# Routed experts turned around: weights stationary, highs and lows of 192 tokens as 384 moving columns

## The chip, the core and the metric

One core of a Trainium2 chip runs the whole program. The metric is device time in microseconds (us) of one execution.

## What is computed

The reference is a chain of three layers in fp32, all in one kernel:

```python
attn = softmax_causal(q k^T / 8 + min(bias, 0)) v        # 2 x 8 heads, 576 tokens, 64 wide
x = attn as 1152 rows of 512
e = argmax(x @ w_gate)                                   # layer 2: one of 8 experts for each row
out[row] = gate[row] * (relu(x[row] @ w1[e]) @ w2[e])    # w1 512x1024, w2 1024x512
out2 = sum over 4 experts of p[:, e] * (relu(out @ u1[e]) @ u2[e])   # layer 3: every row, all 4
```

With these inputs the eight experts of layer 2 get 130, 137, 129, 143, 151, 156, 117 and 189 of the 1152 rows.

## The kernel before

Every large product is made from fp32r operands in three passes: an operand is split into a high part (an fp32r copy, written by ScalarE) and a low part (the fp32 value minus the high), and the sum is high by high, high by low and low by high (`PASSES`). Attention (to 141 us) comes first, then routing, the routed experts (the stage that the change rewrites), a gather, and the dense experts of layer 3.

**Routing.** VectorE makes the one-hot, ranks and slots (L769 to L809). Each expert's rows start at a multiple of 128 in `x_slots` in DRAM. GpSimd scatters the rows there with ten indirect DMAs (L457), reading `slot_of`. Meanwhile TensorE runs 16 matmuls of no use (`keep_clock_wide`, L1091) and makes the first tile directly from `x_nat` with selection matrices (L1101), so that tile does not wait for the scatter.

**Routed stage.** The tile is 128 rows, so the counts above make 15 tiles: two for each expert and one for the expert with 117 rows. In `tile` on TensorE (L1104 to L1153) the tokens are the stationary operand and a weight row of 512 columns moves: 24 matmuls up (L1118), 8 transposes of `h1` (L1126), 24 matmuls down (L1135) and 4 transposes of the next tile's rows (L1085). ScalarE takes ReLU and writes the high parts, VectorE the low parts, scales by the gate (L858), and SyncE stores the tile to `y_slots` (L359).

**Splitting the weights.** The weights of the next expert are split while this one runs. They come in eight pieces of 128 x 1024 through four stages (SyncE, L190); ScalarE writes `w_hi` (L584), VectorE `w_lo` of pieces 0, 1, 2, 4, 5, 6 (L838), and GpSimd that of 3 and 7 (L466). Each stage is loaded again when its low part is done. What orders all of this is each engine's program, in which it stands as it is written.

**Gather and dense stage.** After the last store GpSimd gathers the rows back in token order (L477), TensorE transposes them (L1176) and the others write `x2T` high and low; 6 of the 10 row blocks are transposed inside the first dense expert. Then come 4 experts x 3 chunks of 384 tokens (L1191 up, L1206 down), VectorE adds to `acc` (L910), and SyncE stores `acc` (L390).

Of the kernel before, what the change touches and what calls it, by code (L numbers as in the profile page):

```python
# [26 lines left out]
F32 = mybir.dt.float32  # L27
F32R = mybir.dt.float32r
# [9 lines left out]
NT = 5  # L38
# [26 lines left out]
MAXTILES = N // P  # L65
# [4 lines left out]
def moe_chain_kernel(nc, q, k, v, s, wg, w1, w2, dp, u1, u2, out):  # L70
    x_slots = nc.dram_tensor("x_slots", ((SLOT_TILES + 1) * P, XROW), F32, kind="Internal").ap()
    y_slots = nc.dram_tensor("y_slots", (SLOT_TILES * P, DM), F32, kind="Internal").ap()
# [6 lines left out]
    with ExitStack() as ctx:  # L79
# [10 lines left out]
        gate_now = sb("gate_now", [P, 1], F32)  # L90
# [9 lines left out]
        with ExitStack() as a:  # L100
# [4 lines left out]
            thresholds = sb("thresholds", [P, E1, MAXTILES - 1], F32, a)  # L105
# [37 lines left out]

        with ExitStack() as b:
            x_slot = sb("x_slot", [P, XROW], F32, b)
            xT = [sb(f"xT{c}", [P, KD, P], F32R, b) for c in "hl"]
            h1 = [sb(f"h1_{i}", [P, 512], F32, b) for i in range(2)]
            h1T = [[sb(f"h1T{i}{c}", [P, 4, P], F32R, b) for c in "hl"] for i in range(2)]
            y_sb = sb("y_sb", [P, DM], F32, b)


        x2T = [sb(f"x2T{c}", [P, KD, N], F32R) for c in "hl"]

        acc = sb("acc", [P, RT, DM], F32)
        x2_nat = acc
# [10 lines left out]
            slots_zeroed wg_loaded r_step ex_done onehot_ready rank_ready route_ready first_ready scattered  # L166
            hi_done x_slot_loaded xT_psum xT_hi xT_lo h1_ready relu_done h1T_psum h1T_hi h1T_lo y_ready
            y_scaled y_stored gate_copied y_all_stored x2T_psum x2T_hi x2T_lo h2_psum h2_hi h2_lo y2_ready
            y2_added acc_cleared p2_loaded p2_step out_stored passed y_zeroed pads_zeroed""".split()
# [5 lines left out]

        gathered = [sem(f"gathered{r}") for r in range(RT)]
# [26 lines left out]
        X2_AT = 4  # L203
        X2_WITH = (range(0, 4), range(4, 7), range(7, RT))

        def x2_bank(r):

            return (half[3], bank[2], bank[3], half[0], half[3], bank[2], bank[3], half[3], bank[2], bank[3])[r]
# [57 lines left out]
        def _(sp):  # L266
# [35 lines left out]
            sp.wait_ge(m["consts"], 15)  # L302
# [26 lines left out]
            sp.dma_start(x_slots.rearrange("(t p) c -> p t c", p=P),  # L329
                         zeros[:, :].unsqueeze(1).to_broadcast([P, SLOT_TILES + 1, XROW])).then_inc(m["slots_zeroed"], 16)  # L330

            sp.dma_start(y_slots[LEAST_TILES * P:, :].rearrange("(t p) c -> p t c", p=P),
                         zeros[:, 0:DM].unsqueeze(1).to_broadcast([P, SLOT_TILES - LEAST_TILES, DM])).then_inc(m["y_zeroed"], 16)
            sp.dma_start(p2[:, :, :], dp.rearrange("(t p) e -> p t e", p=P)).then_inc(m["p2_loaded"], 16)
# [9 lines left out]
            sp.wait_ge(m["route_ready"], 2)  # L344
            sp.wait_ge(m["scattered"], 16 * RT)
            sp.dma_start(x_slot[:, :], x_slots[0:P, :]).then_inc(m["x_slot_loaded"], 16)
            sp.wait_ge(m["y_zeroed"], 16)
            sp.sem_inc(m["y_stored"], 16)
            T = sp.alloc_register("sp_tile")
            sp.reg_mov(T, 0)  # L350

            def tile(ge=None, e=None, pieces=(), dense=False):

                t = sp.snap(T, min_val=0, max_val=SLOT_TILES - 1)
                sp.wait_ge(m["gate_copied"], t + 1)
                sp.dma_start(x_slot[:, :], x_slots[bass.ds(t * P + P, P), :]).then_inc(m["x_slot_loaded"], 16)
                stream(ge, e, pieces[:2], dense)
                sp.wait_ge(m["y_scaled"], t + 2)
                sp.dma_start(y_slots[bass.ds(t * P, P), :], y_sb[:, :]).then_inc(m["y_stored"], 16)  # L359
                stream(ge, e, pieces[2:], dense)  # L360
                sp.reg_add(T, T, 1)

            def expert(e, after, after2):


                tile(after[0], after[1], W2S, after[2])
                tiles = sp.value_load(tiles_of[0:1, bass.ds(e, 1)], min_val=1, max_val=MAXTILES)
# [878 lines left out]
```

## Time and profile before

| | |
|---|---|
| median of the timed runs | 790.42 us (788.16, 792.26, 790.42) |
| the profiled execution | 785.49 us, its span 783.3 us |
| granted TensorE clock over the span | 0.989 |
| busy: TensorE, VectorE, ScalarE, GpSimd | 747.8, 321.3, 278.6, 159.7 us |
| routed tiles, from the first matmul to the last | 164.5 to 361.8 us |
| gather and first transposes, to the first dense matmul | 361.8 to 375.6 us |
| dense experts to the end | 375.6 to 783.3 us |

Times in the trace are counted from the start of the span. The busy time of TensorE is a sum of overlapping, modelled durations; the pace of matmuls is read from the distance between their starts.

### The profile page before, as it was taken

The page shows a single profiled execution, that of the slowest core. Times are in us where ns is not written, and L with a number is a line of the kernel's source. Part 1 is how long each engine was busy: PE and PEld are TensorE (multiplying, and loading weights), DVE is VectorE, ACT ScalarE, POOL GpSimd, SP SyncE. Part 2 cuts the span into 40 slices and gives each one's busy share as a digit, 9 for nine tenths or more (in the row PEclk, how much of TensorE's full clock was granted, in tenths as well). Part 3 has the DMA queues.
Part 4 walks back from the last instruction along what each step waited for, and adds up shares of the span by engine and source line. Part 5 has one row for each costly group of instructions (what it writes and reads, how often), then busy time and mean ns, then how long its engine had stood idle before and what let it go on. Part 6 is the DMA issues. An engine that isn't in the chain of part 4 may idle for free.

```text
span 783.3 us, 13131 instructions
## 1 busy us (share of the span) xinstructions
PE 747.8 (95%) x4424; PEld 643.5 (82%) x4425; DVE 321.3 (41%) x800; ACT 278.6 (36%) x620; POOL 159.7 (20%) x174
## 2 busy tenths in 40 slices
PE   6999999799999999979899999999999999999998
PEld 5778777578888778767789999999998989999897
DVE  3777777524545455643452314322133211212122
ACT  3777777034545555543332112311113111111110
POOL 4665675222122121223310000110001100000000
PEclk9999999899999999989999999999999999999999
DMA  7744529246575666666530001310012000001011
GB/s 189 213 109 129 159 71 360 83 130 225 181 240 184 220 204 223 198 219 227 162 108 28 1 1 54 120 41 0 0 28 80 0 0 0 0 0 40 0 40 40
DMA packets 61490, 84.35 MB, mean 108 GB/s; under 512 B 33136, under 2 KB 33136, under 8 KB 60944
## 3 DMA queue, kind: packets, MB, share of 16 engines
q1 hardware_dynamic: 59808, 77.95, 31.7%
q0 software_dynamic: 1472, 4.76, 1.9%
q10 hardware_dynamic: 176, 1.22, 0.4%
q8 instruction: 18, 0.29, 0.1%
q14 instruction: 16, 0.13, 0.1%
HBM read 68.82 MB, written 15.09 MB: 107 GB/s over the span
## 4 chain that ended last, share of the span: by engine, by line
PE 69%; issue 20%; POOL 5%; DMA 2%; SPq 1%; DVE 1%; ACT 1%; POOLq 0%; DVEq 0%; ACTq 0%
PE bank L1191 26%; PE wide L1206 25%; PE bank L1051 4%; POOL w_lo L466 3%; PE bank L1033 3%; PE wide L985 3%; PE bank L1016 2%; DMA stages<-in_moe_w 1%; PE wide L1118 1%; POOL x_slots L457 1%; PE bank L1135 1%; PE wide L990 1%; PE wide L959 1%; SPq L276 1%; DMA acc<-y_slots,slot_of 0%
## 5 line engine op out<-in xcount | busy, mean ns | idle before, releaser
L466 POOL TENSOR_TENSOR w_lo<-stages,w_hi 128x1024 fp32r<-128x1024 f32 x22 | 56.9, 2588 | 379.4 <-ACT w_hi L584 379.4
L1191 PE MATMUL bank<-x2Th,w_hi 128*128 128x384 f32 (+1 forms) x384 | 129.3, 337 | 1.6 <-DVE x2Tl L889 1.6
L1191 PE MATMUL bank<-x2Tl,w_hi 128*128 128x384 f32 (+1 forms) x384 | 129.4, 337 | 0.0
L1191 PE MATMUL bank<-x2Th,w_lo 128*128 128x384 f32 (+1 forms) x384 | 128.9, 336 | 0.0
L584 ACT ACTIVATE w_hi<-stages 128x1024 fp32r<-128x1024 f32 x88 | 89.3, 1051 | 5.0 <-DMA stages<-in_moe_w 5.0
L634 ACT ACTIVATE h_0h<-bank 128x384 fp32r<-128x384 f32 x48 | 23.6, 492 | 188.1 <-PE bank L1191 188.1
L838 DVE TENSOR_TENSOR w_lo<-stages,w_hi 128x1024 fp32r<-128x1024 f32 x66 | 79.7, 1227 | 17.3 <-ACT w_hi L584 16.3
L899 DVE SCALAR_TENSOR_TENSOR h_0l<-bank,h_0h 128x384 fp32r<-128x384 f32 x48 | 26.8, 557 | 142.0 <-ACT h_0h L634 142.0
L899 DVE SCALAR_TENSOR_TENSOR h_1l<-bank,h_1h 128x384 fp32r<-128x384 f32 x48 | 26.7, 557 | 129.1 <-ACT h_1h L634 129.1
L1191 PEld LDWEIGHTS bank<-x2Th,w_hi 128*128 128x128 f32 x384 | 72.1, 188 | 5.5 <-issue 1.9
L1191 PEld LDWEIGHTS bank<-x2Th,w_lo 128*128 128x128 f32 x384 | 72.1, 188 | 3.6
L634 ACT ACTIVATE h_1h<-bank 128x384 fp32r<-128x384 f32 x48 | 23.6, 492 | 140.6 <-PE bank L1191 140.6
L1191 PEld LDWEIGHTS bank<-x2Tl,w_hi 128*128 128x128 f32 x384 | 72.0, 188 | 0.0
L446 POOL TENSOR_TENSOR bias<-cum_bc,cum_col 64x64 f32<-64x64 f32 (+4 forms) x80 | 57.0, 720 | 41.8 <-ACT probs L531 33.9
L1206 PE MATMUL wide<-w_lo,h_0h 128*128 128x512 f32 x144 | 57.0, 396 | 0.0
L1206 PE MATMUL wide<-w_hi,h_0l 128*128 128x512 f32 x144 | 56.9, 395 | 0.0
L1206 PE MATMUL wide<-w_lo,h_1h 128*128 128x512 f32 x144 | 56.7, 394 | 0.0
L1206 PE MATMUL wide<-w_hi,h_1l 128*128 128x512 f32 x144 | 56.6, 393 | 0.0
L1206 PE MATMUL wide<-w_hi,h_1h 128*128 128x512 f32 x144 | 56.2, 390 | 0.0
L1206 PE MATMUL wide<-w_hi,h_0h 128*128 128x512 f32 x144 | 56.0, 389 | 0.0
L1118 PE MATMUL wide<-w_hi,xTh 128*128 128x512 f32 x120 | 48.2, 402 | 2.0 <-DVE xTl L829 1.5
L1118 PE MATMUL wide<-w_hi,xTl 128*128 128x512 f32 x120 | 49.4, 412 | 0.0
(190 smaller groups left out, 1331.6 us busy)
## 6 DMA issues: line engine op xcount, KB each, us to landing
stages<-in_moe_w SPq DMA_DIRECT2D x96, 512.0 KB, 3.8
x_slots<-zeros SPq DMA_DIRECT2D x1, 4420.0 KB, 15.4
x_slot<-x_slots SPq DMA_DIRECT2D x16, 260.0 KB, 3.5
y_slots<-y_sb SPq DMA_DIRECT2D x15, 256.0 KB, 2.6
cum_bc<-cum_dram SPq DMA_DIRECT2D x3, 1152.0 KB, 9.1
out_x<-acc SPq DMA_DIRECT2D x9, 256.0 KB, 2.1
q_nat<-in_q SPq DMA_DIRECT2D x16, 128.0 KB, 2.6
k_nat<-in_k SPq DMA_DIRECT2D x16, 128.0 KB, 4.2
```

The source lines that it names most:

```text
L446: g.tensor_tensor(bias[u % BIASES][0:R, 0:K], cum_bc[0:R, bass.ds((4 * odd + 2 * pl + hh) * S, K)], cum_col[0:R, i, bass.ds(it * 4 + (2 * ...
L466: g.tensor_tensor(w_lo[par][:, c], stage[3][:, :], w_hi[par][:, c].bitcast(F32), ALU.subtract).then_inc(lo_done[3], 1)
L584: sc.activation(w_hi[par][:, u * PIECE:(u + 1) * PIECE], stage[u % 4][:, :], ACT.Copy).then_inc(m["hi_done"], 1)
L634: sc.activation(h2[ft % 2][0][:, :], bank[ft % 2][:, 0:CHUNK], ACT.Relu).then_inc(m["h2_hi"], 1)
L838: ve.tensor_tensor(w_lo[par][:, c], stage[u % 4][:, :], w_hi[par][:, c].bitcast(F32), ALU.subtract).then_inc(lo_done[u % 4], 1)
L899: ve.scalar_tensor_tensor(out=h2[ft % 2][1][:, :], in0=bank[ft % 2][:, 0:CHUNK], scalar=0.0, in1=h2[ft % 2][0][:, :].bitcast(F32), op0=ALU ...
L985: te.matmul(wide[hh][0:R, at:at + a1 - a0], qT[pl][st][rows, c0:c0 + R], kT[pl][mv][rows, a0:a1], start=(n == 0), stop=False, skip_group_c ...
L1033: last = te.transpose(dst, pr[0:R, j * P:(j + 1) * P], ident[0:R, 0:R])
L1051: last = te.matmul(bank[2 + u % 2][h_ * D:(h_ + 1) * D, 0:R], v_nat[pl][:, j, h_ * D:(h_ + 1) * D], pT[h_][u % 2][:, j * R:(j + 1) * R], s ...
L1118: last = te.matmul(half[c], xT[st][:, kk, :], w1_of((w_hi, w_lo)[mv][par], kk, c * 512, 512), start=(n == 0), stop=(n == 11))
L1191: last = te.matmul(bank[ft % 2][:, 0:CHUNK], w1_of((w_hi, w_lo)[st][par], kk, ft * P, P), x_mv, start=(n == 0), stop=(n == 11))
L1206: last = te.matmul(half[o], h2[f % 2][st][:, o * P:(o + 1) * P], w2_of((w_hi, w_lo)[mv][par], f), start=(f == 0 and n == 0), stop=(f == KF ...
```

## The change

- **Weights stationary.** A tile is 192 tokens (`TOK`). Its highs and lows stand side by side in `xT[:, kk, 2, 192]`. For each 128 x 128 block of weights one matmul has the high block stationary and 384 columns moving (highs, then lows), and one has the low block stationary and the 192 highs moving. The product comes out transposed, `h1` with its hidden units on partitions, so `h1` isn't transposed.
- **The two halves are added by VectorE**, with a `tensor_reduce` over a pair 192 columns apart in PSUM: eight of 192 outputs for `h1` and two of 384 outputs for the result in each tile.
- **ScalarE** writes the high of ReLU into `h1T`; **GpSimd** writes ReLU in full and then the low.
- **Splits** stand between these: ScalarE splits piece `ft` behind the ReLU of step `ft`, VectorE piece `ft` behind the sum of step `ft`, GpSimd piece 3 in quarters behind steps 3 to 6 and piece 7 behind step 7.
- **Compact slots.** An expert's rows start where those of the one before end (`off_of`); a tile of 192 may run into the next expert's rows, and its result there is written over by the next tile. With these counts there are 8 tiles.
- **Results stay on chip**, in slot order, as highs and lows in `x2T`; `y_slots`, the gather and its transposes go. The gate is folded into `p2`. The token number and the probabilities travel with the row, and the output is scattered by GpSimd with nine indirect DMAs instead of stored by SyncE.
- **The first tile** is loaded from `x_slots` like the others; 80 matmuls of no use stand ahead of it instead of 16.

```diff
+TOK = 192
+LAG = 3
+RAW = 4
...
@@ tensor
-            keep_clock_wide(16)
-            for r in range(RT):
-                pe.wait_ge(m["first_ready"], r + 1)
...
+            keep_clock_wide(80)
+            turn_x(0)
...
+                def up(ft):
+                    if e is not None and ft == 0:
+                        for kk in range(KD):
                             pe.wait_ge(lo_done[kk], e * 2 + 1)
+                    pe.wait_ge(m["h1_sum"], t * KF + (ft + 1))
+                    for kk in range(KD):
+                        te.matmul(up_bank(ft), w1_of(w_hi[par], kk, ft * P, P), xT[:, kk, :, :].rearrange("p a k -> p (a k)"),
+                                  start=(kk == 0), stop=False, skip_group_check=True)
+                        last = te.matmul(up_bank(ft)[:, 0:TOK], w1_of(w_lo[par], kk, ft * P, P), xT[:, kk, 0, :],
+                                         start=False, stop=(kk == KD - 1), skip_group_check=True)
...
+                for ft in range(KF):
+                    up(ft)
+                    if ft >= LAG:
+                        down(ft - LAG)
+                turn_x(t + 1)
+                for f in range(KF - LAG, KF):
+                    down(f)
@@ vector
+                for ft in range(KF):
+                    dve.wait_ge(m["h1_psum"], t * KF + (ft + 1))
+                    dve.wait_ge(m["h1_lo"], t * KF + (ft + 1))
+                    ve.tensor_reduce(h1[:, ft % RAW, :], up_bank(ft).rearrange("p (a k) -> p k a", a=2), AX.X,
+                                     ALU.add).then_inc(m["h1_sum"], 1)
+                    if split is not None and ft % 4 < 3:
+                        split_lo(*split, ft)
+                x_lo(t + 1)
+                for pr in range(2):
+                    dve.wait_ge(m["x2_psum"], t * 2 + (pr + 1))
+                    ve.tensor_reduce(y1[:, 2 * pr:2 * pr + 2, :], down_pair(pr), AX.X, ALU.add).then_inc(m["x2_sum"], 1)
+                for pr in range(2):
+                    dve.wait_ge(m["x2_hi"], t * 2 + (pr + 1))
+                    ve.tensor_tensor(x2T_part(1, pr, col), ...)
@@ scalar
+                for ft in range(KF):
+                    act.wait_ge(m["h1_sum"], t * KF + (ft + 3))
+                    sc.activation(h1T[:, ft % (LAG + 1), 0, :], h1[:, ft % RAW, :], ACT.Relu).then_inc(m["h1_hi"], 1)
+                    if split is not None and ft < KF - 1:
+                        split_hi(*split, ft)
+                x_hi(t + 1)
+                if split is not None:
+                    split_hi(*split, KF - 1)
@@ gpsimd, in the loop over ft
+                    g.tensor_scalar(r1[:, ft % 2, :], h1[:, ft % RAW, :], 0.0, None, ALU.max).then_inc(m["h1_relu"], 1)
...
+                    g.tensor_tensor(h1T[:, ft % (LAG + 1), 1, :], r1[:, ft % 2, :], h1T[:, ft % (LAG + 1), 0, :].bitcast(F32),
+                                    ALU.subtract).then_inc(m["h1_lo"], 1)
...
+                pool.indirect_dma_start(out[:, :], bass.IndirectOffsetOnAxis(token_of[:, t:t + 1], 0),
+                                        acc[:, t, :], None).then_inc(m["out_stored"], 16)
```

How the instructions stand now, at the two places of which the prediction speaks most. First VectorE, in a routed tile, before the change (`h1T..l` and `xTl` are low parts, `w_lo` the low weights of the next expert):

```order
L846 TENSOR_TENSOR h1T0l<-bank,h1T0h 128x512 [waits h1T_hi]
L838 TENSOR_TENSOR w_lo<-stages,w_hi 128x1024 [waits hi_done]
L846 TENSOR_TENSOR h1T1l<-bank,h1T1h 128x512 [waits h1T_hi]
L852 TENSOR_TENSOR xTl<-wide,xTh 128x512 [waits xT_hi]
L838 TENSOR_TENSOR w_lo<-stages,w_hi 128x1024 [waits hi_done]
L838 TENSOR_TENSOR w_lo<-stages,w_hi 128x1024 [waits hi_done]
L858 TENSOR_SCALAR y_sb<-bank,gate_now 128x512 [waits gate_copied,y_stored]
```

And VectorE in the changed kernel, the first three of eight steps of a tile and then the tile's end (`h` is `h1`, `y` is `y1`):

```order
L883 TENSOR_REDUCE h<-bank 128x192 [waits h1_psum,h1_lo]
L873 TENSOR_TENSOR w_lo<-stages,w_hi 128x1024 [waits hi_done]
L883 TENSOR_REDUCE h<-bank 128x192 [waits h1_psum,h1_lo]
L873 TENSOR_TENSOR w_lo<-stages,w_hi 128x1024 [waits hi_done]
L883 TENSOR_REDUCE h<-bank 128x192 [waits h1_psum,h1_lo]
...
L890 TENSOR_REDUCE y<-wide 128x384 [waits x2_psum]
L890 TENSOR_REDUCE y<-wide 128x384 [waits x2_psum]
L893 ISA [waits x2_hi]
L893 TENSOR_TENSOR x2Tl<-y,x2Th 128x2x192
```

Where one weight split stood between three pieces of a tile's own work, a split now stands behind each of six sums, so the next sum is issued only when the split ahead of it has been.

Second ScalarE in the changed kernel, the first steps of a tile:

```order
L661 ACTIVATE h1T<-h 128x192 [waits h1_sum]
L654 ACTIVATE w_hi<-stages 128x1024 [waits stage_full0]
L661 ACTIVATE h1T<-h 128x192 [waits h1_sum]
L654 ACTIVATE w_hi<-stages 128x1024 [waits stage_full1]
L661 ACTIVATE h1T<-h 128x192 [waits h1_sum]
L654 ACTIVATE w_hi<-stages 128x1024 [waits stage_full2]
```

Before, each ReLU was followed by a copy of its transpose, and a split stood alone between them or three together at the tile's end; now each high of the weights stands behind a ReLU that waits for VectorE's sum.

## Rows read from the trace of the kernel before

**Rows 1.** Windows: busy us (x instructions) of PE, PEld, DVE, ACT, POOL; clock; DMA; GB/s.
```profile
164.50:327.90 163.40, 163.23 (x780) 130.85 (x781) 83.67 (x103) 88.11 (x118) 32.18 (x12) 1.00 0.62 200
```

**Rows 2.** Chain of waits, routed stage (start us, us, what).
```profile
177.11 2.67 POOL w_lo L466
...
189.64 2.67 POOL w_lo L466
```

**Rows 3.** Timeline of TensorE: dense matmuls (384 columns), then fp32 transposes (128).
```profile
773.47 0.34 PE L1191 MATMUL bank<-x2Th,w_lo 128*128 x1
773.64 0.34 PE L1191 MATMUL bank<-x2Tl,w_hi 128*128 x1
...
64.87 0.27 PE L959 MATMUL wide<-ident,q_nat 128*128 128x128 f32 x1
64.98 0.27 PE L960 MATMUL wide<-ident,k_nat 128*128 128x128 f32 x1
```

**Rows 4.** Groups by line and form: the splits.
```profile
L584 ACT ACTIVATE w_hi<-stages 128x1024 fp32r<-128x1024 f32 x88 | 89.3, 1051 | 5.0 <-DMA stages<-in_moe_w 5.0
L564 ACT ACTIVATE w_hi<-stages 128x512 fp32r<-128x512 f32 x8 | 5.1, 636 | 0.6 <-DMA stages<-in_moe_w 0.6
L838 DVE TENSOR_TENSOR w_lo<-stages,w_hi 128x1024 fp32r<-128x1024 f32 x66 | 79.7, 1227 | 17.3 <-ACT w_hi L584 16.3 <-issue 1.0
```

**Rows 5.** Groups by line and form: VectorE from PSUM, and its strided reductions.
```profile
L899 DVE SCALAR_TENSOR_TENSOR h_0l<-bank,h_0h 128x384 fp32r<-128x384 f32 x48 | 26.8, 557 | 142.0 <-ACT h_0h L634 142.0
L769 DVE TENSOR_REDUCE r_lg<-head_logits 128x80 f32<-128x640 f32 x1 | 1.3, 1296 | 0.0
L788 DVE TENSOR_REDUCE e_cnt<-r_one 128x8 f32<-128x80 f32 x1 | 0.3, 294 | 0.0
```

**Rows 6.** Groups by line and form: GpSimd.
```profile
L466 POOL TENSOR_TENSOR w_lo<-stages,w_hi 128x1024 fp32r<-128x1024 f32 x22 | 56.9, 2588 | 379.4 <-ACT w_hi L584 379.4
L430 POOL TENSOR_TENSOR w_lo<-stages,w_hi 128x256 f32 x32 | 23.5, 735 | 7.9 <-ACT w_hi L564 7.8
L446 POOL TENSOR_TENSOR bias<-cum_bc,cum_col 128x192 f32<-128x192 f32 x16 | 8.1, 507 | 15.2 <-ACT probs L531 15.2
```

**Rows 7.** Timeline, all engines: how close two instructions follow each other.
```profile
168.98 0.60 ACT L592 ACTIVATE h1T0h<-bank 128x512 fp32r<-128x512 f32 x1 [0.78 <-PE bank L1126]
169.47 1.05 ACT L584 ACTIVATE w_hi<-stages 128x1024 fp32r<-128x1024 f32 x1
170.55 1.23 DVE L838 TENSOR_TENSOR w_lo<-stages,w_hi 128x1024 fp32r<-128x1024 f32 x1 [0.26 <-ACT w_hi L584]
175.16 2.36 DVE L838 TENSOR_TENSOR w_lo<-stages,w_hi 128x1024 fp32r<-128x1024 f32 x2 [0.25 <-ACT w_hi L584]
```

**Rows 8.** Timeline of VectorE: first instruction behind a tile's end, past its branches.
```profile
330.40 1.43 DVE L838 TENSOR_TENSOR w_lo<-stages,w_hi 128x1024 fp32r<-128x1024 f32 x1 [1.00 <-issue]
```

**Rows 9.** Timeline: TensorE's matmuls of no use; the first and tenth scatter.
```profile
146.92 6.39 PE L1091 MATMUL bank<-w_hi 128*128 128x512 f32 x16
149.79 1.11 POOL L457 DMA_INDIRECT x_slots<-x_nat,slot_of  x1 [15.86 <-DVE tiles_of L809]
...
161.50 0.97 POOL L457 DMA_INDIRECT x_slots<-x_nat,slot_of  x1 [0.30 <-issue]
```

**Rows 10.** DMA issues (KB each, median us to landing).
```profile
stages<-in_moe_w SPq DMA_DIRECT2D x96, 512.0 KB, 3.8
x_slot<-x_slots SPq DMA_DIRECT2D x16, 260.0 KB, 3.5
...
out_x<-acc SPq DMA_DIRECT2D x9, 256.0 KB, 2.1
...
x_slots<-x_nat,slot_of POOLq DMA_INDIRECT x10, 2.7
```

**Rows 11.** Windows around a pause of TensorE (columns as in rows 1).
```profile
332.70:337.70 5.00, 0.00 (x1) 0.01 (x1) 1.88 (x2) 2.60 (x3) 0.47 (x1) 0.89 1.00 351
337.70:340.00 2.30, 2.30 (x8) 2.01 (x9) 0.52 (x1) 1.15 (x2) 1.90 (x1) 0.50 0.54 219
```

More of the change, by code:

```diff
@@ L200, in moe_chain_kernel, with up_bank, down_bank, down_pair @@
         PASSES = ((0, 0), (1, 0), (0, 1))
[L203 to L208, printed above, removed]
+        def up_bank(ft):
+            return bank[ft % 2][:, 0:2 * TOK]
+        def down_bank(dt):
+            return half[dt][:, 0:2 * TOK]
+        def down_pair(pr):
+            banks = wide[pr][:, :].rearrange("p (c k) -> p c k", c=2)[:, :, 0:2 * TOK]
+            return banks.rearrange("p c (a k) -> p c k a", a=2)
+        TURN_ROWS = (P, TOK - P)
+        def tile_start(off, j):
+            return nc.s_assert_within(off + j * TOK, 0, N, skip_runtime_bounds_check_because="a tile that is run starts at a row of its expert")
+        def turn_bank(g):
+            return bank[2 + g][:, 0:KD * TURN_ROWS[g]].rearrange("p (c r) -> p c r", c=KD)
+        def xT_part(hl, g):
+            return xT[:, :, hl, g * P:g * P + TURN_ROWS[g]]
+        def x2T_part(hl, pr, col):
+            flat = x2T[hl][:, 2 * pr:2 * pr + 2, :]
+            return flat[:, :, bass.ds(col, TOK)]
         def alone(eng):
@@ L384, in _ @@
+            expert(E1 - 1, 0, (E1, 0, True), (E1 + 1, 1, True))
             stream(E1 + 1, 1, W2S, True)
@@ new lines, in _ @@
+            with dve.Fori(0, E1 // 2) as pair:
+                e0 = pair * 2
+                for par in range(2):
+                    e = e0 + par
+                    tiles = dve.value_load(tiles_of[0:1, bass.ds(e, 1)], min_val=1, max_val=MAXT)
+                    off = dve.value_load(off_of[0:1, bass.ds(e, 1)], min_val=0, max_val=N)
+                    tile(off, (e + 1, 1 - par))
+                    with dve.If(tiles > 1):
+                        with dve.Fori(1, MAXT) as j:
+                            with dve.If(j < tiles):
+                                tile(tile_start(off, j))
@@ L1080, in _ @@
                       skip_group_check=True).then_inc(m["rank_ready"], 1)
-            def transpose_x():
-                for c in range(KD):
-                    last = te.transpose(half[3][:, c * P:(c + 1) * P], x_slot[:, c * P:(c + 1) * P], ident[:, :])
-                last.then_inc(m["xT_psum"], 1)
             def keep_clock_wide(times):
@@ new lines, in down @@
+                def down(f):
+                    if e is not None and f % 2 == 0:
+                        pe.wait_ge(lo_done[f // 2], e * 2 + 2)
+                    pe.wait_ge(m["h1_lo"], t * KF + (f + 1 + RAW))
+                    if f == 0:
+                        pe.wait_ge(m["x2_sum"], t * 2 + 2)
+                    for dt in range(KD):
+                        w_rows = [w2_of(w[par], f)[:, dt * P:(dt + 1) * P] for w in (w_hi, w_lo)]
+                        te.matmul(down_bank(dt), w_rows[0], h1T[:, f % (LAG + 1), :, :].rearrange("p a k -> p (a k)"),
+                                  start=(f == 0), stop=False, skip_group_check=True)
+                        last = te.matmul(down_bank(dt)[:, 0:TOK], w_rows[1], h1T[:, f % (LAG + 1), 0, :],
+                                         start=False, stop=(f == KF - 1), skip_group_check=True)
+                        if f == KF - 1 and dt % 2 == 1:
+                            last.then_inc(m["x2_psum"], 1)
@@ L1194, in dense_chunk @@
                         last.then_inc(m["h2_psum"], 1)
-                    if ft == X2_AT and first is not None:
-                        with pe.If(first):
-                            for r in X2_WITH[c + 1]:
-                                transpose_x2(r)
                     if ft >= 1:
```

438 lines of the change are left out of this document (176 added, 262 removed).

## The prediction

> **What bounds the kernel now.** I read the windows first. In the stretch of the routed stage where every expert has two tiles, TensorE is busy for 163.23 of 163.40 us at full clock, VectorE for 83.67 and ScalarE for 88.11 [rows 1]: it is bound by TensorE, and the others have half their time free. The chain of waits shows GpSimd's split once in every tile, but its rows serve as a ruler only: 12.5 us from one to the next, the length of a tile [rows 2]. The timeline of TensorE gives its pace. A 384-column matmul starts 0.17 to 0.18 us after the one before, and the 128-column transposes 0.11 us apart [rows 3]; so a matmul with a weight load of its own costs 0.457 ns a column, and not under about 0.11 us. Beside 48 matmuls of 512 columns a tile has 12 transposes, and 15 tiles fill 164.5 to 361.8 us.
>
> **TensorE after the change.** A tile has 64 pairs of one 384- and one 192-column matmul. The long one costs 0.175. The short one, which no row shows, costs between 0.088 (by its columns) and 0.11 (the transposes); I take 0.11, since each has its own weight load. 64 x 0.285 = 18.2 us and eight transposes 0.9 make 19.1 us, against 25.1 for the two tiles that it replaces. If TensorE still set the pace, 8 tiles would take 153 us in place of 197. It won't, I think.
>
> **The chain that replaces it.** The order of VectorE and ScalarE closes a ring. Sum `ft+1` stands behind VectorE's split of piece `ft`, that waits for ScalarE's high of piece `ft`, that stands behind the ReLU of step `ft`, and that waits for sum `ft`. One turn of it:
>
> - The sum, 384 values in and 192 out, read from PSUM at a stride. No row shows one. The contiguous PSUM row of 384 is 0.557. The strided reductions of the trace (in SBUF) take 1.296 for 640 values and 0.294 for 80 [rows 5], so 1.79 ns a value, 0.84 for 384; the contiguous rows of VectorE give 1.05 ns a value (0.557 for 384, 1.227 for 1024) [rows 4, 5]. I take 0.84, since the pair of one sum lies 192 columns apart.
> - The hand-over to ScalarE 0.03 and its ReLU: 0.636 for 512 and 1.051 for 1024 [rows 4] give 0.377 for 192. The next instruction there starts some 0.10 before its end [rows 7], so 0.28.
> - ScalarE's high of a piece 1.05 and a hand-over 0.03 [rows 4, 7].
> - VectorE's low of the piece, 1.13 until its next instruction starts (two take 2.36) [rows 7].
>
> That is 3.36 us, while TensorE needs 2.28 for one up and one down. LAG and the two PSUM banks don't help: TensorE is ahead already. GpSimd's work in a turn is its ReLU (0.51, the 192-wide row), the low (2.41 ns a value between 256 and 1024, so 0.58) and at most a quarter 0.735 [rows 6]: 1.8 us, hidden.
>
> **One tile**, from its first sum: sums 0 to 3 start at 0, 3.36, 6.72, 10.08. Piece 3 is GpSimd's, so sum 4 follows at 10.8, but ScalarE works through two ReLUs and two highs and sum 5 comes at 14.7; sum 6 at 18.0, sum 7 at 21.4, done at 22.2. GpSimd's ReLU and low end at 23.4, and TensorE's last down gives the first half of the result 0.9 later, at 24.3. Two sums of 768 (1.53 each at 1.79 ns; 0.96 contiguous) end at 27.3, ScalarE's high of 384 (0.53) at 27.8. VectorE's last low starts there, and then come the loop's branches and two register loads. The one place where such a passage is bare shows 1.0 us of idle time behind a 0.15 copy [rows 8]; so the next sum starts 1.15 after the low did, at **29.0**. Beside this runs piece 7: GpSimd's last quarter of piece 3 at 20.8, a load of 3.8 [rows 10] and its issue, ScalarE's high by 26.1. It is hidden by 1.2 us, and would come to light if the sums were cheap.
>
> **The stage.** The scatter starts with slots that are ready some 0.6 us sooner (three short steps fewer ahead of them), and takes its 11.7 us to the tenth issue and 2.7 to land, so it is done at 163.6 [rows 9, 10]. The rows' load, 3.5 and two issues of 0.35 [rows 10], now stands ahead of the first tile: 167.4. 80 matmuls of no use reach to 167.8: 16 take from 146.9 to 153.3 [rows 9], and 64 more of 512 columns 14.6 at 0.457 ns a column. Transposes, highs and lows take it to 170.4 and the first sum starts at 171.8. Seven tiles of 29.0 and the eighth to its end, where GpSimd's low of piece 7 is last (29.3), bring the first dense matmul to 404.0. Before it was 375.6, and the gather and its transposes were in that. This is +28.4.
>
> **The rest.** Dense stage: 24 transposes go, at 0.11 [rows 3], -2.6. The end: an indirect store lands 2.7 after its issue instead of 2.1, and three of them queue at 1.3 us each on GpSimd behind sums that come every 0.75 [rows 9, 10], +1.7. The zeroed `y_slots`, the stores and the token and probability loads lie beside other work, nothing. **Sum: +27.5, so 813 against the profiled execution's 785.5.** That execution was 4.9 under the median of the timed runs, so I forecast 790.4 + 27.5 = **818 us**.
>
> **The two rules.** With the stride priced as a contiguous read the turn would be 3.07. The Trainium skill, VectorE: DVE Perf Modes, section Mode 1× (REGULAR) — the baseline, says that this mode takes fp32, odd strides and PSUM operands alike at one result a cycle, and its section The perf-mode tier table gives `tensor_reduce` no other mode; by this the sum would be the cheap one and the forecast the first rival. Against it stands the Trainium skill, SBUF — State Buffer, in the note on cachelines in its section Door 1: The DMA port swizzle: lines are 16 bytes in SBUF and 8 in PSUM, and each access that crosses to a new one pays. The rows at a stride bear it out for SBUF with 1.79 against 1.05 ns; for PSUM no row here shows it.
>
> **Rivals.**
> - *The stride costs nothing.* For it: the strided rows are SBUF. Sums 0.56 and 0.96; a tile loses seven times 0.28 and twice 0.57, and piece 7's load then takes 0.9 back: 26.8 us, 801 in all, 796 with the passage between tiles hidden. Chance 0.22.
> - *TensorE stays the bound, faster.* If splits don't hold up the sums (they run in VectorE's idle time, because ScalarE is ahead), a tile costs 19.1 and the dense stage starts 77 us sooner than in my sum: 741. It wins from under about 25 us a tile. For it: VectorE and ScalarE together have time enough (some 18 and 13 us of work a tile). Against it: the order of the two, in which nothing can be passed, and rows for the splits with 88 and 66 samples. 0.09.
> - *The stride in PSUM costs more than in SBUF.* At 3 ns a value the sum is 1.3: 34 us a tile, 858. 0.08.
> - *TensorE's clock falls at tile ends.* It pauses for near 3 us there. After a pause of 5 us it was granted 0.50 [rows 11], the 1.2 GHz level; in attention, with short pauses, it kept 2.4. Two steps with up and down would then take 4.6 in place of the ring's 3.36: 2.4 a tile, 837. 0.09.
> - *No change,* between: cheap stride and a little off each step. 0.05.
>
> **How the numbers follow.** My case has 0.47. The likeliest time is 818. The range reaches down to the cheap stride with its passage hidden, 796, and up to near the dear stride, 856; 0.14 lie below and 0.04 above. About 0.5% is what a measurement of this kernel can tell from no change; faster by over that has 0.09, within it 0.05, slower 0.86.
>
> **What would show it.** In the changed kernel's trace: TensorE idle for about a third of the routed stage, waiting for L883 or for what hangs on it; the first sums of a tile 3.4 us apart (3.1 in the first rival, under 2.5 in the second); L883 at 0.84 mean; tiles 29 us apart; the short matmuls 0.11 after the long ones; the first dense matmul near 404. It would be wrong if L873 never waited for L654 for long, or if tiles came less than 25 us apart.

## The result, and the profile after

The changed kernel takes **823.35 us** (median of 4 runs, 822.48 to 823.70) against 791.34 for the kernel before on the same chip (4 runs, 788.16 to 794.31): ratio 1.040, 95% interval 1.036 to 1.045. Forecast were 818 and slower, with a range of 796 to 856. The profiled execution took 823.7, with a span of 821.7.

The page of the changed kernel: its span, the busy time of each engine, and in 40 slices TensorE's and its clock.

```profile
span 821.7 us, 13995 instructions
PE 734.2 (89%) x4532; PEld 657.0 (80%) x4533; DVE 343.3 (42%) x820; ACT 264.7 (32%) x632; POOL 264.6 (32%) x351
PE   6999988876967877986699999999999999999996
PEclk9999999899879988888999999999999999999999
```

In slices 9 to 20, the routed stage, TensorE's row is mostly at 6 to 8, and in seven of them the clock stands at 7 or 8. The window from the first up matmul nearly to the last (busy us of PE, PEld, DVE, ACT, POOL, then clock, DMA share and GB/s):

```profile
170.60:400.00 229.40, 179.08 (x1063) 167.94 (x1064) 124.28 (x152) 93.51 (x154) 141.42 (x184) 0.88 0.47 149
```

Against [rows 1], where TensorE was busy for 163.23 of 163.40, it now stands idle for 50.3 of 229.4 us, and GpSimd works for 62% of the time in place of 20%. What TensorE waited for from 170.6 to 411.5 us (us in total, times, longest), from the waits:

```profile
PE bank L1137 <- DVE h L883: 29.5, 18, 3.0
PE wide L1151 <- POOL h1T L516: 13.1, 16, 1.2
PE bank L1137 <- issue: 8.8, 6, 6.6
PE bank L1190 <- POOL w_lo L501: 5.9, 1, 5.9
```

The first line is the wait that was forecast. The second (GpSimd's low of h1, not ready for the down matmul) and most of the third weren't. The fourth is the wait for the last piece's low, which the forecast held in its last tile. The groups of the instructions that the prediction priced:

```profile
L873 DVE TENSOR_TENSOR w_lo<-stages,w_hi 128x1024 fp32r<-128x1024 f32 x66 | 84.9, 1286 | 78.4 <-ACT w_hi L654 78.4
L516 POOL TENSOR_TENSOR h1T<-r,h1T 128x192 fp32r<-128x192 f32 x64 | 56.1, 876 | 13.4 <-POOL r L512 13.4
L512 POOL TENSOR_SCALAR r<-h 128x192 f32<-128x192 f32 x64 | 43.8, 685 | 58.1 <-DVE h L883 57.6
L883 DVE TENSOR_REDUCE h<-bank 128x192 f32<-128x384 f32 x64 | 34.6, 548 | 12.0 <-PE bank L1139 7.5 <-issue 4.5
L890 DVE TENSOR_REDUCE y<-wide 128x384 f32<-128x768 f32 x16 | 14.7, 953 | 9.4 <-PE wide L1153 9.3
L893 DVE TENSOR_TENSOR x2Tl<-y,x2Th 128x384 f32 x16 | 14.1, 921 | 9.0 <-ACT x2Th L669 9.0
```

The sum of 384 values takes 0.548 us and not 0.84: it costs what the contiguous row of [rows 5] costs, and its larger sister 0.953 for 768. VectorE's split takes 1.286, above the 1.227 of [rows 4], and the low of h1 0.876 where 0.58 was expected. The 78.4 us that L873 waited for L654 are the ring (the chain of waits that the prediction draws from one sum of `h1` to the next) at work. VectorE's timeline in one tile shows its turn (start, us, instruction, idle time before it):

```profile
234.89 0.56 DVE L883 TENSOR_REDUCE h<-bank 128x192 f32<-128x384 f32 x1 [4.92 <-PE bank L1139]
236.82 1.39 DVE L873 TENSOR_TENSOR w_lo<-stages,w_hi 128x1024 fp32r<-128x1024 f32 x1 [1.38 <-ACT w_hi L654]
238.13 0.55 DVE L883 TENSOR_REDUCE h<-bank 128x192 f32<-128x384 f32 x1
240.06 1.39 DVE L873 TENSOR_TENSOR w_lo<-stages,w_hi 128x1024 fp32r<-128x1024 f32 x1 [1.38 <-ACT w_hi L654]
241.37 0.55 DVE L883 TENSOR_REDUCE h<-bank 128x192 f32<-128x384 f32 x1
```

One turn of the ring, from sum to sum, is 3.24 us: 0.59 from the sum to ScalarE's ReLU, 0.27 to its split, 1.07 to VectorE's split, 1.31 to the next sum. In the second half of the same tile it is 3.07, where VectorE's split takes 1.23 and the next sum comes 1.14 behind it. GpSimd there:

```profile
246.25 0.60 POOL L516 TENSOR_TENSOR h1T<-r,h1T 128x192 fp32r<-128x192 f32 x1 [0.21 <-POOL r L512]
...
250.97 1.52 POOL L516 TENSOR_TENSOR h1T<-r,h1T 128x192 fp32r<-128x192 f32 x1 [0.21 <-POOL r L512]
252.45 0.72 POOL L501 TENSOR_TENSOR w_lo<-stages,w_hi 128x256 fp32r<-128x256 f32 x1
253.15 0.68 POOL L512 TENSOR_SCALAR r<-h 128x192 f32<-128x192 f32 x1
254.04 1.51 POOL L516 TENSOR_TENSOR h1T<-r,h1T 128x192 fp32r<-128x192 f32 x1 [0.21 <-POOL r L512]
```

The same low takes 0.60 in an early turn and 1.51 in a late one, where it meets VectorE's split. From 250.97 to 254.04 GpSimd needs 3.07 us for a turn in which 1.8 had been forecast. It has no slack left: there are two loops of one length here, and the ring is only one of them. This trace doesn't say what GpSimd's would be without the ring, since its low ends 0.45 behind VectorE's split in each late turn; experiment 2 does.

### The profile page after: what moved, and what is told of

It reads as the page before. It is cut to its first block, busy times and chain, and to the rows that moved or that the text cites. A ratio compares the mean times of both kernels' runs of the same rounds, so it can differ in the third digit from the quotient of the medians.

```text
span 821.7 us, 13995 instructions
## 1 busy us (share of the span) xinstructions
PE 734.2 (89%) x4532; PEld 657.0 (80%) x4533; DVE 343.3 (42%) x820; ACT 264.7 (32%) x632; POOL 264.6 (32%) x351
## 3 DMA queue, kind: packets, MB, share of 16 engines
q10 hardware_dynamic: 176, 1.22, 0.4%
## 4 chain that ended last, share of the span: by engine, by line
PE 69%; issue 12%; POOL 6%; DVE 4%; ACT 2%; SPq 1%; DMA 1%; DVEq 1%; POOLq 0%; ACTq 0%
PE bank L1190 25%; PE wide L1201 24%; PE bank L1074 4%; POOL r L512 3%; PE bank L1056 3%; PE wide L1008 3%; PE bank L1109 2%; DVE h L883 2%; PE bank L1137 2%; POOL w_lo L501 2%; ACT w_hi L654 2%; DMA stages<-in_moe_w 1%; PE bank L1039 1%; PE wide L1151 1%; POOL h1T L516 1%
## 5 line engine op out<-in xcount | busy, mean ns | idle before, releaser
L1137 PE MATMUL bank<-xT,w_hi 128*128 128x384 f32 x256 | 91.4, 411 | 40.1 <-DVE h L883 29.5
L873 DVE TENSOR_TENSOR w_lo<-stages,w_hi 128x1024 fp32r<-128x1024 f32 x66 | 84.9, 1286 | 78.4 <-ACT w_hi L654 78.4
L654 ACT ACTIVATE w_hi<-stages 128x1024 fp32r<-128x1024 f32 x88 | 92.1, 1047 | 26.4 <-DMA stages<-in_moe_w 26.4
L1151 PE MATMUL wide<-h1T,w_hi 128*128 128x384 f32 x256 | 86.0, 389 | 13.1 <-POOL h1T L516 13.1
L1137 PEld LDWEIGHTS bank<-xT,w_hi 128*128 128x128 f32 x256 | 55.1, 215 | 46.3 <-DVE h L883 34.3
L487 POOL TENSOR_TENSOR w_lo<-stages,w_hi 128x1024 fp32r<-128x1024 f32 x6 | 14.4, 2393 | 221.5 <-ACT w_hi L654 221.5
L1139 PE MATMUL bank<-xT,w_lo 128*128 128x192 f32 x256 | 69.6, 272 | 0.0
L1153 PE MATMUL wide<-h1T,w_lo 128*128 128x192 f32 x256 | 66.9, 261 | 0.0
L1151 PEld LDWEIGHTS wide<-h1T,w_hi 128*128 128x128 f32 x256 | 51.8, 202 | 17.3 <-POOL h1T L516 16.8
L512 POOL TENSOR_SCALAR r<-h 128x192 f32<-128x192 f32 x64 | 43.8, 685 | 58.1 <-DVE h L883 57.6
L543 POOL DMA_INDIRECT out_x<-acc,token_of x9 | 8.8, 974 | 162.1 <-DVE acc L937 160.9
```

Source lines behind the costliest of these rows:

```text
L512: g.tensor_scalar(r1[:, ft % 2, :], h1[:, ft % RAW, :], 0.0, None, ALU.max).then_inc(m["h1_relu"], 1)
L654: sc.activation(w_hi[par][:, u * PIECE:(u + 1) * PIECE], stage[u % 4][:, :], ACT.Copy).then_inc(m["hi_done"], 1)
L873: ve.tensor_tensor(w_lo[par][:, c], stage[u % 4][:, :], w_hi[par][:, c].bitcast(F32), ALU.subtract).then_inc(lo_done[u % 4], 1)
L1137: te.matmul(up_bank(ft), w1_of(w_hi[par], kk, ft * P, P), xT[:, kk, :, :].rearrange("p a k -> p (a k)"), start=(kk == 0), stop=False, skip ...
L1139: last = te.matmul(up_bank(ft)[:, 0:TOK], w1_of(w_lo[par], kk, ft * P, P), xT[:, kk, 0, :], start=False, stop=(kk == KD - 1), skip_group_c ...
L1151: te.matmul(down_bank(dt), w_rows[0], h1T[:, f % (LAG + 1), :, :].rearrange("p a k -> p (a k)"), start=(f == 0), stop=False, skip_group_ch ...
```

## The experiments

Each ratio is to runs of the kernel before on the same chip; the changed kernel's own is 1.040 (1.036 to 1.045). The kernel before took 791.34 us beside the changed kernel and 786.9 to 787.4 beside the experiments, so a difference from the changed kernel is uncertain by some 4 us. The start of the dense stage in the traces (411.4 us in the changed kernel) is given where it says more.

**1. The sum done twice.** Doubles one link of the ring.

```diff
+                    ve.tensor_reduce(twice[:, ft % RAW, :], up_bank(ft).rearrange("p (a k) -> p k a", a=2), AX.X, ALU.add)
                     ve.tensor_reduce(h1[:, ft % RAW, :], up_bank(ft).rearrange("p (a k) -> p k a", a=2), AX.X,
                                      ALU.add).then_inc(m["h1_sum"], 1)
```

> The changed kernel with each h1 sum made twice (64 more reductions; the first goes to a buffer that nothing reads). Ring theory (sum, ReLU, ScalarE split, VectorE split follow one another in every step): each step of a tile grows by the issue distance of a sum, 0.45 us, in 7 of 8 steps, so 3.2 us a tile and 25 us in all, about 848. If GpSimd sets steps 4 to 6 as closely as the ring does, these absorb part of it: 12 to 18 us. If the sums are off the critical path (TensorE or the tile ends set the time): 0 to 3 us.

Measured: 847.11 us, ratio 1.076 (1.073 to 1.079), some 0.036 or 28 us above the changed kernel; the dense stage starts at 433.4, 22 later. The sums now start 3.70 apart where it was 3.24 (240.87, 244.57, 248.27 in its timeline). 0.46 us more on VectorE, which is idle for 1.38 us of every turn, goes into the time nearly in full: 22 to 28 us where 25 were forecast by the ring and 12 to 18 if GpSimd set the later steps. The ring theory holds, and idle time of the engine is no slack.

**2. Only the order on VectorE.** Sum `ft+1` is issued ahead of the split of piece `ft`.

```diff
-                    if split is not None and ft % 4 < 3:
-                        split_lo(*split, ft)
+                    if split is not None and ft > 0 and (ft - 1) % 4 < 3:
+                        split_lo(*split, ft - 1)
```

> The changed kernel with one thing moved: on VectorE the split of piece ft stands behind the sum of step ft+1 instead of ahead of it. Ring theory: the ring is open, VectorE needs 1.7 us a step and ScalarE 1.3, TensorE's 2.3 sets the pace, and a tile falls from 29.9 to 21 to 23 us: 765 to 775. GpSimd theory (its ReLU, its low drawn out to 1.5 us beside VectorE's split, and a quarter split make 3.05 us a step in steps 4 to 6): steps 0 to 2 get shorter, steps 3 to 6 stay near 3.0, a tile 26 to 27 us: 795 to 802.

Measured: 806.18 us, ratio 1.024 (1.021 to 1.026): 13 us gained (the dense stage starts at 393.6, 18 sooner), less than either theory said. The waits of this kernel, 170 to 394 us, TensorE's first, and then GpSimd's timeline in one tile:

```profile
PE wide L1151 <- POOL h1T L516: 15.5, 18, 2.0
PE bank L1137 <- DVE h L883: 15.4, 6, 2.8
...
DVE w_lo L873 <- ACT w_hi L654: 11.3, 11, 2.2
...
ACT w_hi L654 <- DMA stages<-in_moe_w: 61.1, 15, 7.9
```

```profile
241.49 1.66 POOL L512 TENSOR_SCALAR r<-h 128x192 f32<-128x192 f32 x1
243.35 1.47 POOL L516 TENSOR_TENSOR h1T<-r,h1T 128x192 fp32r<-128x192 f32 x1 [0.21 <-POOL r L512]
244.79 0.73 POOL L501 TENSOR_TENSOR w_lo<-stages,w_hi 128x256 fp32r<-128x256 f32 x1
245.49 1.69 POOL L512 TENSOR_SCALAR r<-h 128x192 f32<-128x192 f32 x1
```

VectorE's wait for ScalarE's split falls from 71.4 us in the routed stage of the changed kernel to 11.3, so the ring is open; TensorE's 18 waits for VectorE are 6, each at a tile's end. But GpSimd's low still comes late: a turn of its loop takes up to 4.00 us (241.49 to 245.49), with nothing idle but the 0.21 ahead of its low. The next tile's first sum comes 11.4 to 13.9 us behind the last one, where the changed kernel has 8.8 to 9.5 (the pause at the second tile's end left out of both). ScalarE now waits 61.1 us for pieces whose stage GpSimd frees late. GpSimd's loop took the ring's place at once.

**3. Only GpSimd relieved.** VectorE takes the low of h1 in one operation behind its split; GpSimd keeps the quarters of pieces 3 and 7.

```diff
...
+                    ve.scalar_tensor_tensor(out=h1T[:, ft % (LAG + 1), 1, :], in0=h1[:, ft % RAW, :], scalar=0.0,
+                                            in1=h1T[:, ft % (LAG + 1), 0, :].bitcast(F32), op0=ALU.max, op1=ALU.subtract)
```

> The changed kernel with GpSimd's ReLU and low of h1 replaced by one scalar_tensor_tensor on VectorE, which stands behind the split of its step; GpSimd keeps only pieces 3 and 7. Ring theory: the ring stays closed and gets 0.3 us longer by that operation but 0.15 shorter by undisturbed splits, and the end of the tile gains 1.5 us since the last low no longer queues on GpSimd: 815 to 830, no great change. GpSimd theory: a tile falls to 26 us or less, under 795.

Measured: 821.33 us, ratio 1.042 (1.040 to 1.045), no change. A turn is 3.34 us there (sums at 237.49, 240.83, 244.17): VectorE's split is back at 1.23 with GpSimd out of its way, and the low adds 0.27 to the ring. The next tile's first sum comes 7.0 behind the last one instead of 9.0, and the longer turns take that back. Without GpSimd's loop the ring still holds the time; the theory that GpSimd is the bound by itself is out.

**4. ScalarE's highs of x2 ahead of its split of piece 7.**

```diff
-                if split is not None:
-                    split_hi(*split, KF - 1)
                 for pr in range(2):
                     act.wait_ge(m["x2_sum"], t * 2 + (pr + 3))
                     sc.activation(x2T_part(0, pr, col), y1[:, 2 * pr:2 * pr + 2, :], ACT.Copy).then_inc(m["x2_hi"], 1)
+                if split is not None:
+                    split_hi(*split, KF - 1)
```

> The changed kernel with ScalarE's two highs of the result ahead of its split of piece 7, instead of behind it. In the changed kernel's trace that split waits 3.4 us for the load of piece 7 and the result waits behind it for 1.3 us. If this holds the tile's end up: 1.3 us a tile and 8 to 11 us in all, about 813. If TensorE's restart holds it up rather than VectorE: 0 to 3 us.

Measured: 818.86 us, ratio 1.040 (1.038 to 1.042): no change by the ratios, but the traces show a gain. The first sums of tiles are 28.2 to 28.6 us apart (33.2 at the second) where the changed kernel has 28.9 to 29.7 (33.5), 0.8 us less in the mean, and the first dense matmul comes at 405.4 instead of 411.4; the turns in between are the same 3.24 and 3.07. So the late high did hold the tile's end, for less than the 1.3 us forecast. In the changed kernel it stands behind ScalarE's split of piece 7, which waits 3.3 us for its load; the prediction says that this load would come to light if the sums were cheap, and its first rival puts it at 0.9.

**5. Both of 2 and 3 together.** The low of block `ft-1` and the split of piece `ft-1` stand behind sum `ft`, both on VectorE.

```diff
-                    if split is not None and ft % 4 < 3:
-                        split_lo(*split, ft)
+                    if ft > 0:
+                        h1_low(t, ft - 1)
+                    if split is not None and ft > 0 and (ft - 1) % 4 < 3:
+                        split_lo(*split, ft - 1)
+                h1_low(t, KF - 1)
```

> Both changes of the two runs before together: VectorE takes the lows of h1 itself, in one operation a block (0.42 us in the third run) that stands behind the next block's sum, and pieces follow behind it; GpSimd keeps only the eight quarters of pieces 3 and 7. VectorE then has 0.55 + 0.42 + 1.25 = 2.2 us a step and waits for nothing of GpSimd's; TensorE has 2.3 us a step. Ring theory (the step is the chain sum, handover, ReLU, ScalarE's split, handover, VectorE's split): the chain is open, a tile comes near TensorE's 19.1 us plus the turn at its end, 22 to 24 us, the kernel 770 to 785 us. GpSimd theory: in the second run GpSimd alone held the time, so with it relieved the same 770 to 785 us. Load theory (the load of piece 7, whose stage is freed by GpSimd's last quarter of piece 3, holds each tile): the quarters of piece 3 no longer wait for h1, so the stage is freed early and the gain is all there; if the loads themselves are the bound (4 MB an expert), a tile cannot be under about 26 us and the kernel stays at 795 to 805 us.

Measured: **774.18 us, ratio 0.985 (0.982 to 0.988)**: 1.5% faster than the kernel before. 2 alone gained 13 us and 3 nothing, but together they give 0.055 of the ratio, 43 us: two loops of one length, each of which hides what opening the other is worth. VectorE's timeline:

```profile
175.71 0.55 DVE L878 TENSOR_REDUCE h<-bank 128x192 f32<-128x384 f32 x1
176.18 0.35 DVE L867 SCALAR_TENSOR_TENSOR h1T<-h,h1T 128x192 fp32r<-128x192 f32 x1
176.45 1.22 DVE L862 TENSOR_TENSOR w_lo<-stages,w_hi 128x1024 fp32r<-128x1024 f32 x1
177.58 0.55 DVE L878 TENSOR_REDUCE h<-bank 128x192 f32<-128x384 f32 x1
```

The turn is 1.87 us with nothing idle in it, until VectorE has caught up with TensorE, and 2.28 from there on. What is left of TensorE's waits is at the tiles' ends, from 170 to 365 us:

```profile
PE bank L1135 <- DVE h L878: 15.2, 6, 2.8
PE bank L1135 <- issue: 3.7, 1, 3.7
PE bank L1188 <- DVE x2Tl L891: 3.3, 1, 3.3
PE bank L1135 <- DVE xT L850: 1.8, 1, 1.8
```

From number 2 to this one the routed stage shrinks by 36 us (223.0 to 187.4): 22 us are idle time of TensorE, and 14 its busy time, as its clock over the stage rises from 0.90 to 0.95. Piece 3's stage is freed early here too (ScalarE's waits for loads fall from 61.1 to 3.6 us), as it was in number 3 without a gain. No run parts this from GpSimd's late low, so the load theory is ruled out only in its second half, that the loads themselves hold the tile at 26 us: tiles are 22.3 to 24.2 us apart here.

**6. Number 5 with the order of number 4.**

> The kernel of the run before (e4_both), and on ScalarE the highs of x2 stand ahead of the split of piece 7, as in the run with that order alone, which changed nothing while the ring and GpSimd set the step. If the wait of ScalarE for piece 7's load now ends each tile, this gains 1 to 2 us a tile, 8 to 15 us on the run before; if VectorE or the loads set the tile, nothing (within 3 us).

Measured: 775.61 us, ratio 0.985 (0.983 to 0.987): nothing, as for a tile that VectorE's end holds. ScalarE's waits for loads grew from 3.6 to 16.6 us.

**7. The lows of x2 moved into the next tile,** behind its first sum, with the column kept in a register (initial and last lows outside the loop).

```diff
                 for ft in range(KF):
+                    if ft == 1:
+                        x2_lows(t)
...
-                for pr in range(2):
-                    dve.wait_ge(m["x2_hi"], t * 2 + (pr + 1))
-                    ve.tensor_tensor(x2T_part(1, pr, col), ...)
```

> The kernel with both changes (e4_both), and VectorE's two lows of x2 moved out of the end of a tile to behind the next tile's first sum, where VectorE waits for TensorE (0.60 us idle between the first two sums in e4_both). At each tile's end e4_both's TensorE stands 2.42 us waiting for that first sum, behind two sums of y, two highs on ScalarE and two lows. If that chain is what holds the first sum, 1.1 us of lows and their wait of some 0.5 us for the high go from it: 1.5 us a tile, seven tiles, 10 us, the kernel 760 to 768 us, ratio 0.965 to 0.977. Rival: the loads of an expert (4 MB) or the split of piece 7 hold the tiles as soon as they get shorter than 23 us; then it stays within 3 us of e4_both.

Measured: **754.18 us, ratio 0.959 (0.955 to 0.963)**, 20 us better than number 5 where 10 were expected, and outside the range given. TensorE's waits, 165 to 375 us:

```profile
PE bank L1147 <- issue: 3.8, 1, 3.8
PE bank L1200 <- DVE x2Tl L880: 3.3, 1, 3.3
PE bank L1147 <- DVE h L892: 2.9, 6, 0.7
```

The wait at the tiles' ends is down from 15.2 to 2.9 us. The two profiled executions are 16.5 us apart (number 5's was the fastest of its four). Of that, TensorE's idle time in the stage gives 12.6 and its busy time 3.7 (164.8 to 161.0), as its clock there rises from 0.95 to 0.98 without the pauses. TensorE now sets the stage: from its first up matmul at 170.44 to the dense stage at 341.47 it is busy for 161.01 of 171.03 us.

**8. What distance costs a reduction.** Eight reductions of 384 values ahead of the first tile: pairs 192 apart (far), pairs side by side (near), eight values 8 apart (row), eight side by side (one); `s` from SBUF, `p` from PSUM.

```diff
+            for where, t_ in (("s", cum_bc[:, 0:384]), ("p", bank[0][:, 0:384])):
+                ve.tensor_reduce(f_[where + "far"][:, :], t_.rearrange("p (a k) -> p k a", a=2), AX.X, ALU.add)
+                ve.tensor_reduce(f_[where + "near"][:, :], t_.rearrange("p (k a) -> p k a", a=2), AX.X, ALU.add)
...
```

> Eight added reductions of 384 values on VectorE, alone, between the routing and the first tile, their results unused: pairs 192 values apart (the form of the changed kernel's sum), pairs side by side, eight values 8 apart and eight values side by side, each once from SBUF and once from PSUM. Theory of the prediction (the reduce of the routing's sum over heads took 4.4 ns a value because its values are 8 apart in SBUF): the 8-apart form takes over 2.5 ns a value from SBUF and the side-by-side forms 1.0 to 1.4. Rival, nothing is paid for distance in either memory: all forms of one memory take the same, 0.45 to 0.6 us. Rival, it is the number of values per result or the count of short rows: both eight-value forms are dear, whether side by side or apart.

(The 4.4 in this text is a slip: 1.296 us for 640 values [rows 5] is 2.0 ns a value.) The groups by line and form:

```profile
L859 DVE TENSOR_REDUCE f_srow<-cum_bc 128x48 f32<-128x384 f32 x1 | 0.8, 845 | 0.0
...
L857 DVE TENSOR_REDUCE f_sfar<-cum_bc 128x192 f32<-128x384 f32 x1 | 0.6, 554 | 0.0
L857 DVE TENSOR_REDUCE f_pfar<-bank 128x192 f32<-128x384 f32 x1 | 0.5, 547 | 0.0
L861 DVE TENSOR_REDUCE f_pone<-bank 128x48 f32<-128x384 f32 x1 | 0.5, 547 | 0.0
L859 DVE TENSOR_REDUCE f_prow<-bank 128x48 f32<-128x384 f32 x1 | 0.5, 546 | 0.0
L858 DVE TENSOR_REDUCE f_pnear<-bank 128x192 f32<-128x384 f32 x1 | 0.5, 545 | 0.0
L858 DVE TENSOR_REDUCE f_snear<-cum_bc 128x192 f32<-128x384 f32 x1 | 0.5, 542 | 0.0
L861 DVE TENSOR_REDUCE f_sone<-cum_bc 128x48 f32<-128x384 f32 x1 | 0.5, 541 | 0.0
```

One form of eight is dear: values 8 apart in SBUF, 845 ns against 541 (2.2 ns a value, less than the 2.5 expected). From PSUM all four cost the same, and pairs 192 apart are cheap in both memories. So the rows that priced the sum were right for their own form, and that form wasn't the sum's.

**9. GpSimd and VectorE side by side.** GpSimd's part of the addition; VectorE's is one operation in a loop beside it.

```diff
...
+                for n in range(4):
+                    if k < 4:
+                        last = g.tensor_tensor(g_out[k][:, :], ga, gb, ALU.subtract)
+                    else:
+                        last = g.tensor_scalar(g_out[4][:, :], ga, 0.0, None, ALU.max)
...
```

> Added ahead of the first tile, results unused: GpSimd's subtraction of 192 values (the form of its low of h1) four times alone, then four times while VectorE runs subtractions of 1024 values with both inputs in SBUF (the form of its split), four times beside reductions of 384 values from PSUM, four times beside one-input operations of 1024 values in SBUF, and GpSimd's one-input operation of 192 values four times beside the subtractions of 1024. Theory, from the changed kernel's trace (0.59 us alone, 1.51 us where it starts while a split runs): an SBUF operation of VectorE with two inputs holds GpSimd's back; alone 0.5 to 0.6 us, beside the subtractions 0.9 to 1.6 us, beside the reductions from PSUM as alone. Rival, GpSimd's long ones were due to something else of that moment (its own handovers, the loads into SBUF): all four the same, 0.5 to 0.6 us. VectorE's own subtractions of 1024 values: 1.23 us alone and 1.35 to 1.4 us beside GpSimd's, by the two levels that the split has in the changed kernel.

GpSimd's groups, window by window: its subtraction alone; beside VectorE's subtractions of 1024 from SBUF; beside its reductions from PSUM; beside its one-input operations from SBUF; and last GpSimd's own one-input operation beside subtractions:

```profile
L490 POOL TENSOR_TENSOR g_out<-cum_bc 128x192 f32<-128x192 f32 x4 | 2.4, 598 | 2.2 <-DMA x_slots<-x_nat,slot_of 1.9
...
L490 POOL TENSOR_TENSOR g_out<-cum_bc 128x192 f32<-128x192 f32 x4 | 6.0, 1500 | 0.4 <-POOL g_out L490 0.2
...
L490 POOL TENSOR_TENSOR g_out<-cum_bc 128x192 f32<-128x192 f32 x4 | 2.4, 588 | 2.8 <-DVEq L885 2.6
...
L490 POOL TENSOR_TENSOR g_out<-cum_bc 128x192 f32<-128x192 f32 x4 | 3.8, 952 | 4.9 <-DVEq L885 4.6
...
L492 POOL TENSOR_SCALAR g_out<-cum_bc 128x192 f32<-128x192 f32 x4 | 5.3, 1315 | 1.8 <-DVEq L885 1.5
```

And VectorE's subtractions in the second of these windows, least, median and most of the line:

```profile
L873 DVE TENSOR_TENSOR v_out<-cum_bc x6: 1224/1494/1497, 166.3 to 173.7; 128x1024 f32<-128x1024 f32 x6
```

0.60 alone, 1.50 beside two-input subtractions from SBUF, 0.59 beside reductions from PSUM; the theory holds. VectorE pays too: 1.49 against 1.22, more than the 1.35 to 1.40 expected. Its one-input operation from SBUF holds GpSimd up as well (0.95), which the theory, with two inputs only, left out.

## Why the prediction was right, and where its terms were off

The direction and the mechanism came out, and the range held the time: 823.35 against 818. That the time is so near is in part luck. The sum of +27.5 was counted on the profiled execution, and the spans of the two profiled executions are 38.4 us apart (783.3 and 821.7), 10.9 more than forecast; put on the median of the kernel before, 4.9 above its profiled execution, the same sum misses by 5.3. Point by point:

- *TensorE's pace.* A pair of a 384- and a 192-column matmul takes 0.285 us, as forecast, though not in the parts that were forecast: the next matmul starts 0.20 behind a long one and 0.09 behind a short one, instead of 0.175 and 0.11 (starts 343.78, 343.87 and 344.07 in number 5); the two misses cancel. Once the ring is open the turns take 2.28 us (323.54 to 325.82 there), the forecast pace of TensorE. Number 7 runs at 754 where that rival said 741.
- *The ring.* Right, and tested: 1 lengthens it and the time follows; 3 shows that it holds without GpSimd; 5 removes it. Its price was 3.36 and is 3.24 and 3.07. **The sum was mis-sized**, 0.548 in place of 0.84, since its stride was priced by SBUF rows of another form (number 8). The Trainium skill, VectorE: DVE Perf Modes, section Mode 1× (REGULAR) — the baseline, has odd strides and PSUM operands work in this mode at its one result a cycle; that they cost no more agrees with both rows of the sum and seven of the eight forms, but the time goes by values read and not by results (0.548 us for 384 in and 192 out, 0.953 for 768 in and 384 out). The note on cachelines in the Trainium skill, SBUF — State Buffer, section Door 1: The DMA port swizzle, has each access that crosses to a new line pay. That agrees with the eighth form, 845 against 541 ns, and neither with the PSUM ones, 546 against 547, nor with pairs 192 apart in SBUF, 554 against 542.
- *VectorE's split* was taken at 1.13 to the next instruction and is 1.31 in the early turns, beside GpSimd. This gave 0.18 of the 0.29 back.
- *GpSimd hidden, 1.8 us a turn.* **Wrong**: 3.07 in the late turns, and 13.1 us of TensorE's waits are for it. The durations were read alone, and added; contention wasn't in the sum (number 9). In the changed kernel as it stands this costs little, because the ring is as long. It is what made number 2 fall short.
- *One tile.* 29.0 forecast. First sums of tiles are 29.2, 33.5, 29.1, 29.7, 29.1, 29.5 and 28.9 us apart. The last sum of a tile came at 20.1 instead of 21.4, but the first of the next 9.0 behind it instead of 7.6: the sums of y start 4.1 behind it and not 2.9, since GpSimd's last low is late; they take 2.02 instead of 3.06; the lows of x2 and the passage to the next tile 2.4 instead of 1.2. The high that waits behind piece 7 is some 0.8 of this (number 4). Cheap sums, and dear contention with a piece 7 that isn't hidden, came out even: a right total from wrong terms, and so luck.
- *The pause that no term held*: 33.5 is the second tile. At the first return of the expert loop TensorE stands for 6.64 us with no releaser but "issue", and runs at half clock (0.50) for the next 5.0. Cost: 4.5 us against the forecast tile.
- *The stage* ends at 411.35 instead of 404.0: 0.4 before the first sum, 4.5 for the pause, 1.5 in the other six tiles, 0.8 in the last.
- *Dense and end.* From the first dense matmul to the last 402.57, before 403.70: -1.1, not -2.6. The stage now starts behind 5.9 us of idle time at a clock of 0.82 over its first 10 us, and it was 1.00 before. From the last matmul to the end of the span 7.78 against 4.00: +3.8, not +1.7. With the stage's 7.4 these misses, 1.5 and 2.1, make up the 10.9.
- *The rivals.* The cheap stride was true as a fact and wrong as a time (801): what it saved, contention, the pause and the dense stage's start and end took. TensorE became the bound only with the edits of number 5 and, at the tiles' ends, of number 7. The clock did fall, as the fourth rival says: at the start of every tile from the second on, 10 us at a mean of 0.53 to 0.83. It hardly cost a thing: the turns there are 3.23 or 3.24 as elsewhere. The first three steps have up matmuls alone, half the work that the rival's 4.6 us was made of.

What stays open is the cause of the pause at the loop's first return. Every version has it there, under "issue" or GpSimd's split as its releaser. It is 5.5 to 6.6 us long where GpSimd makes the lows of h1 and 3.7 to 4.2 where it doesn't, and no run varied the loop's code.

## What to carry to other kernels

When an engine is busy for about half of a stage (VectorE here for 124 of 229 us) and still sets its time, follow one instruction around: a chain of waits that closes through the issue order of two engines has a length of its own, and it is cut by issuing the next producer ahead of work that waits. Before saying "hidden", add up each neighbour's loop with durations from where it will run, beside the others; when two loops are of one length, an edit to one shows little or nothing (13 and 0 us here), and only both together do (43). Price an access form by rows of the same form and memory.

## What the runs showed of the hardware

- A reduction of 384 fp32 values takes 0.54 to 0.55 us in seven of eight forms (all four from PSUM, 8 or 192 apart or side by side), and 0.845 with values 8 apart in SBUF.
- GpSimd's operations on SBUF are held up by VectorE's on SBUF: 0.60 becomes 1.50 us beside two-input ones, 0.95 beside one-input ones, and stays 0.59 beside reductions from PSUM. VectorE's two-input ones go from 1.22 to 1.49. GpSimd's one-input operation, 0.69 in the early turns of the changed kernel, takes 1.32 beside VectorE's two-input ones, which stay at 1.24. The Trainium skill, SBUF — State Buffer, section SBUF: two separate sides, calls the shared port pair an exclusive lock, also for VectorE's operations with two SBUF inputs; that GpSimd waits agrees. That whoever holds it keeps it for its whole instruction doesn't agree in full: the two alternated every 1.50 us, and 1.22 + 0.60 would be 1.82.
- Behind a 192-column matmul, with a weight load of its own, the next starts 0.09 us later where it stands between 384-column ones. 128-column transposes one behind another are 0.11 apart [rows 3].
